# Attention with the values as weights: two output tiles side by side on TensorE, divided by spread inverse row sums on VectorE

## The reference, cut to what matters

```python
# q, k, v: (4 batches, 8 heads, 576, 64)
scores = scale * q @ k.T
thresh = max(scores, axis=-1) - tau
attn   = exp(where(scores >= thresh, scores, -1e9) - max)
attn   = attn / (sum(attn, axis=-1) + 1e-9)
x      = attn @ v                       # heads are joined: x is (4, 576, 512)
# part 2 ("dense" in the kernel), per batch
x_prev = x shifted by one row
xk, xr = mu_k*x + (1-mu_k)*x_prev, mu_r*x + (1-mu_r)*x_prev
x2     = sigmoid(xr @ w_r) * (relu(xk @ w_k)**2 @ w_v)
u      = x2 + real(fft(fft(x2, axis=1), axis=2))
# part 3, over all 2304 rows
out    = u + relu(norm(u) @ w_ch1) @ w_ch2
```

## Time and profile before

| | |
|---|---|
| median of 3 runs | 1061.82 us (1059.22 to 1061.85) |
| the profiled execution | 1060.8 us, its span 1059.0 us |
| granted TensorE clock over the span | 1.00 |
| attention with set-up, nothing beside it | 0 to about 110 us |
| attention with part 2 of the batch before beside it | about 110 to 565 us |
| part 2 of the last batch alone | about 565 to 700 us |
| part 3 | about 700 to 1059 us |

### The profile page before, as it was taken

How to read it: one execution, slowest core, us unless ns; L and a number is a source line. 1 busy time by engine, 2 the same in 40 slices (tenths; PEclk the granted TensorE clock), 3 DMA queues, 4 the chain that set the end, 5 groups by cost and what they waited for, 6 DMA issues and landing times.

```text
span 1059.0 us, 18200 instructions
## 1 busy us (share of the span) xinstructions
PE 1031.8 (97%) x6896; PEld 980.0 (93%) x6896; DVE 580.2 (55%) x1135; ACT 504.4 (48%) x1252; POOL 415.7 (39%) x363
## 2 busy tenths in 40 slices
PE   6899899999999999999999999999999999999998
PEld 6898899999899999999999999888888888888998
DVE  6998995467875467874565687443214214114111
ACT  5989785656775647775647653211111111111110
POOL 4888784334664434573423246331211211111000
PEclk9999999999999999999999999999999999999999
DMA  8736112023302032301023137101001000100000
GB/s 237 203 88 192 45 45 58 3 90 118 102 27 59 1 121 87 105 25 37 20 94 111 45 123 276 41 1 64 9 1 37 36 1 34 38 1 1 36 1 35
DMA packets 41271, 70.08 MB, mean 66 GB/s; under 512 B 6624, under 2 KB 22368, under 8 KB 40672
## 3 DMA queue, kind: packets, MB, share of 16 engines
q1 hardware_dynamic: 40880, 68.59, 20.6%
q10 hardware_dynamic: 304, 0.33, 0.1%
HBM read 56.50 MB, written 12.41 MB: 65 GB/s over the span
## 4 chain that ended last, share of the span: by engine, by line
PE 84%; POOL 5%; DVE 4%; ACT 4%; issue 2%; DMA 0%; SPq 0%; DVEq 0%; POOLq 0%; ACTq 0%
PE PB L840 21%; PE PB L841 21%; PE PB L842 21%; PE PB L906 8%; PE PB L867 6%; PE PB L886 5%; PE PB L908 1%; DVE probs L1443 1%; DVE neg_s L1432 1%; ACT exps L1163 1%; POOL wkl L705 1%; POOL k_lo L696 1%; POOL q_hl L689 1%; ACT mix_v L1235 1%; ACT probsT L1172 1%
## 5 line engine op out<-in xcount | busy, mean ns | idle before, releaser
L1389 ACT ACTIVATE h_hi<-PB 128x464 fp32r<-128x464 f32 (+1 forms) x80 | 44.5, 556 | 329.7 <-PE PB L842 329.7
L1676 DVE SCALAR_TENSOR_TENSOR h_lo<-PB,h_hi 128x464 fp32r<-128x464 f32 (+1 forms) x80 | 51.0, 638 | 256.7 <-ACT h_hi L1389 256.7
L1443 DVE SCALAR_TENSOR_TENSOR probs<-neg_s,thresh,exps 128x576 f32<-128x576 f32 x144 | 158.9, 1104 | 1.6 <-ACT exps L1163 1.3
L906 PE MATMUL PB<-v_sb,probsT 128*128 128x64 f32 (+1 forms) x1152 | 145.9, 270 | 0.0
L906 PEld LDWEIGHTS PB<-v_sb,probsT 128*128 128x128 f32 x1152 | 140.6, 193 | 0.0
L1432 DVE TENSOR_SCALAR_CACHE_REDUCE neg_s<-PB,taus 128x576 f32<-128x576 f32 x144 | 116.9, 812 | 42.5 <-PE PB L867 38.7
L1172 ACT ACTIVATE probsT<-PB 128x256 f32<-128x256 f32 (+1 forms) x288 | 103.5, 414 | 73.2 <-PE PB L886 72.6
L842 PE MATMUL PB<-un_h,w1l 128*128 128x464 f32 (+1 forms) x320 | 118.8, 371 | 0.0
L841 PE MATMUL PB<-h_lo,w2h 128*128 128x464 f32 (+1 forms) x320 | 118.8, 371 | 0.0
L840 PE MATMUL PB<-h_hi,w2h 128*128 128x464 f32 (+1 forms) x320 | 118.8, 371 | 0.0
L842 PE MATMUL PB<-h_hi,w2l 128*128 128x464 f32 (+1 forms) x320 | 118.8, 371 | 0.0
(11 more groups left out here) (204 smaller groups left out, 2432.5 us busy)
## 6 DMA issues: line engine op xcount, KB each, us to landing
q_raw<-qT_dram SPq DMA_DIRECT2D x62, 160.0 KB, 3.1
k_raw<-kT_dram SPq DMA_DIRECT2D x64, 144.0 KB, 3.2
w_raw<-w_dram SPq DMA_DIRECT2D x8, 1024.0 KB, 8.1
u_scr<-x2T SPq DMA_DIRECT2D x4, 1152.0 KB, 4.8
cd<-cd_scr SPq DMA_DIRECT2D x4, 1032.0 KB, 5.0
v_sb<-v_dram SPq DMA_DIRECT2D x16, 256.0 KB, 3.2
u_in<-u_scr SPq DMA_DIRECT2D x4, 928.0 KB, 5.1
out_dram<-u_in SPq DMA_DIRECT2D x16, 232.0 KB, 2.1
```

The lines of the kernel that those rows point to most:

```text
L906: last = nc.tensor.matmul(both[:, own], probsT[:, n % 2, kt * P128:(kt + 1) * P128], v_sb[:, kt, pair % 2, own], start=jj in (0, TAIL) and ...
L1443: nc.vector.scalar_tensor_tensor(probs[:, n % 2, place_of(n):place_of(n) + S], neg_s[:, n % 2, :], thresh[:, col:col + 1], exps[:, n % 2, ...
L1676: nc.vector.scalar_tensor_tensor(h_lo[:, ft % 3, 0:w], bank(4 + ft % 3)[:, 0:w], 0.0, h_hi[:, ft % 3, 0:w].bitcast(F32), ALU.max, ALU.subt ...
```

## The change

- `pv` works on groups: two full tiles of a head, or the mixed tile, or the two last; five groups a pair (slots `jj` 1, 3, 4, 6, 8). The head's values (64 columns) are now the weights, the transposed probabilities move (128 columns). The two tiles of a group go to partitions 0 to 63 and 64 to 127 of one bank, by two matmuls behind each other (`both_halves`). Outputs have channels on the partitions.
- Since rows of queries are now along the free axis, the inverse row sums can't be a scale any more. `spread` lets TensorE multiply `rowinv`, broadcast to 64 columns as weights, with the identity, so that they lie along the free axis on 64 partitions: five pairs of matmuls for a pair of heads. ScalarE copies them to `inv_rows` (`copy_inverse`, two copies a pair), and VectorE multiplies outputs by them into `x_att` (`mixed_out`, one instruction a pair; `tiles_out`, four).
- ScalarE's ten `copy_tile` copies a pair and TensorE's 20 transposes a batch are gone. `xT` is filled from `x_att` in SBUF, by four copies of 576 columns a batch.
- `pv` comes ahead of `transpose_probs` in a slot. The ring of PSUM banks has no groups "x" any more.
- `gate_alone` moves to another place in SBUF.

```diff
+GROUP_OF = (0, 0, 1, 1, 2, 3, 3, 4, 4)
+GROUP_ENDS = {1: 0, 3: 1, 4: 2, 6: 3, 8: 4}
...
+                def both_halves(out, first, second, start, stop):
+                    for half, (weights, moving) in enumerate((first, second)):
+                        last = nc.tensor.matmul(out[half * DH:(half + 1) * DH, :], weights, moving, start=start, stop=stop)
+                    return last
+
+                def spread(pair, tiles, cols):
+                    weights = [rowinv[:, pair % 2, t:t + 1].broadcast_to([P128, DH]) for t in tiles]
+                    moving = [ident[:, :], ident[:, :]] if tiles[0] != tiles[1] else [ident[:, 0:DH], ident[:, DH:P128]]
+                    return both_halves(beside_outputs(pair)[:, cols], (weights[0], moving[0]), (weights[1], moving[1]), True, True)
+
+                def pv_mixed(pair):
...
+                    for kt in range(KT):
+                        weights = [v_sb[:, kt, pair % 2, h * DH:(h + 1) * DH] for h in range(2)]
+                        moving = [probsT[:, n % 2, kt * P128 + h * DH:kt * P128 + (h + 1) * DH] for h in range(2)]
+                        last = both_halves(beside_outputs(pair)[:, 0:DH], (weights[0], moving[0]), (weights[1], moving[1]), kt == 0, kt == KT - 1)
+                    last.then_inc(pv_ready, 1)
+                    pe.wait_ge(inv_ready, pair * 2 + 1)
+                    spread(pair, (TAIL, TAIL), slice(DH, 2 * DH))
+                    for g in range(2):
+                        last = spread(pair, (2 * g, 2 * g + 1), slice(2 * DH + g * P128, 2 * DH + (g + 1) * P128))
+                    last.then_inc(spread_ready, 1)
...
                 def pv(n):
...
                     for kt in range(KT - 1):
-                        last = nc.tensor.matmul(both[:, own], probsT[:, n % 2, kt * P128:(kt + 1) * P128], v_sb[:, kt, pair % 2, own], start=jj in (0, TAIL) and kt == 0, stop=False)
-                    if jj >= TAIL:
-                        last = nc.tensor.matmul(both, probsT[:, n % 2, (KT - 1) * P128:KT * P128], v_sb[:, KT - 1, pair % 2, :], start=False, stop=jj in (TAIL, TILES_PAIR - 1))
+                        weights = v_sb[:, kt, pair % 2, own]
+                        moving = [probsT[:, t % 2, kt * P128:(kt + 1) * P128] for t in tiles]
+                        last = both_halves(outputs(pair)[:, place], (weights, moving[0]), (weights, moving[1]), jj == 1 and kt == 0, False)
+                    if h == 1:
+                        moving = [probsT[:, t % 2, (KT - 1) * P128:KT * P128] for t in tiles]
+                        for head in range(2):
+                            weights = v_sb[:, KT - 1, pair % 2, head * DH:(head + 1) * DH]
+                            place = slice((2 * head + g) * P128, (2 * head + g + 1) * P128)
+                            last = both_halves(outputs(pair)[:, place], (weights, moving[0]), (weights, moving[1]), False, jj == TILES_PAIR - 1 and head == 1)
                     last.then_inc(pv_ready, 1)
+                    if jj == TILES_PAIR - 1:
+                        pe.wait_ge(inv_ready, pair * 2 + 2)
+                        pe.wait_ge(x_out, pair * 5 + 1)
+                        for g in range(2):
+                            last = spread(pair, (TILES_PAIR - 1 - 2 * g, TILES_PAIR - 2 - 2 * g), slice(2 * DH + g * P128, 2 * DH + (g + 1) * P128))
...
                 def dense(d):
-                    for dt in range(DT):
...
-                        for st in range(FULL):
-                            last = nc.tensor.transpose(ring(d, "x", 0, dt)[:, st * P128:(st + 1) * P128], x_att[:, st, dt * P128:(dt + 1) * P128], ident[:, :])
...
+                    if 0 <= n - 4 < TILES:
+                        pv(n - 4)
                     if 0 <= n - 3 < TILES:
                         transpose_probs(n - 3)
-                    if 0 <= n - 4 < TILES:
-                        pv(n - 4)
...
-                def copy_tile(pair, i):
...
+                def copy_inverse(pair, second):
+                    act.wait_ge(spread_ready, pair * 2 + second + 1)
...
+                    nc.scalar.activation(inv_rows[:, to], beside_outputs(pair)[:, source], ACT.Copy).then_inc(inv_copied, 1)
...
-                        nc.scalar.activation(xT[:, dt, 1:FULL * P128 + 1], ring(d, "x", 0, dt), ACT.Copy).then_inc(xt_copied_a, 1)
+                        nc.scalar.activation(xT[:, dt, 1:S + 1], x_att[:, dt, :], ACT.Copy).then_inc(xt_copied_a, 1)
...
+                def mixed_out(pair):
...
+                    nc.vector.tensor_tensor(x_att[:, dt, FULL * P128:S], beside_outputs(pair)[:, 0:DH], inv_rows[:, 0:DH], ALU.mult).then_inc(x_out, 1)
+
+                def tiles_out(pair, h):
...
+                    for odd in range(2):
...
+                        nc.vector.tensor_tensor(to[:, :, odd, :], some[0], some[1], ALU.mult).then_inc(x_out, 1)
...
+                    for at, out_of in ((9, mixed_out), (13, lambda pair: tiles_out(pair, 0)), (14, lambda pair: tiles_out(pair, 1))):
+                        heads, rest = divmod(n - at, TILES_PAIR)
```

More of the change, by code:

```diff
@@ L189, in bank_turns @@
 def bank_turns():
-    order = [(0, "x", 0, i) for i in range(5)]
+    order = []
     for d in range(B):
@@ L207, in bank_turns @@
         d, stage = group[:2]
-        if alone(d) and stage != "x":
+        if alone(d):
             of[group] = next(six)
@@ L211, in bank_turns @@
             of[group] = 4
-        elif alone(d) or (drains(d) and stage == "u"):
+        elif drains(d) and stage == "u":
             of[group] = next(four)
@@ L452, in ring, with outputs, beside_outputs @@
             return bank(BANK_OF[d, stage, c, i])
-        def outputs(pair, i):
-            at = 0 if i == TAIL else i * 2 * DH
-            return bank(6 + (pair + (i == TAIL)) % 2)[:, at:at + 2 * DH]
+        def outputs(pair):
+            return bank(6 + pair % 2)
+        def beside_outputs(pair):
+            return bank(6 + (pair + 1) % 2)
         def mean_out(c):
@@ L898, in pv @@
+                def pv(n):
+                    jj, pair = n % TILES_PAIR, n // TILES_PAIR
+                    if jj not in GROUP_ENDS:
+                        return
+                    if jj == TAIL:
+                        pv_mixed(pair)
+                        return
+                    h, g = half_of(n), row_of(n) // 2
+                    if jj == 1:
                         pe.wait_ge(v_in[pair % 2], 48 * (pair // 2) + 48)
-                    if n == 0:
-                        pe.wait_ge(v_padded, 1)
+                        if pair == 0:
+                            pe.wait_ge(v_padded, 1)
+                        else:
+                            pe.wait_ge(inv_copied, pair * 2)
@@ L901, in pv @@
                     pe.wait_ge(unit_copied, 2 * n + 2)
-                    both = outputs(pair, i)
-                    own = slice(0, 2 * DH) if jj == TAIL else slice(p * DH, (p + 1) * DH)
+                    tiles = (n - 1, n) if h == 0 else (n, n - 1)
+                    own = slice(h * DH, (h + 1) * DH)
+                    place = slice((2 * h + g) * P128, (2 * h + g + 1) * P128)
                     for kt in range(KT - 1):
-                        last = nc.tensor.matmul(both[:, own], probsT[:, n % 2, kt * P128:(kt + 1) * P128], v_sb[:, kt, pair % 2, own], start=jj in (0, TAIL) and kt == 0, stop=False)
@@ L919, in mean @@
                         pe.wait_ge(mean_set, 1)
+                        pe.wait_ge(x_out, B * PAIRS * 5)
                     if c > 0:
@@ L1375, in _ @@
                         copy_units(n - 2)
-                    pair, at = divmod(n - 10, TILES_PAIR)
-                    if 0 <= pair < B * PAIRS:
-                        for i in COPIED_AT.get(at, ()):
-                            copy_tile(pair, i)
+                    for second, at in enumerate((7, 11)):
+                        pair, rest = divmod(n - at, TILES_PAIR)
+                        if rest == 0 and 0 <= pair < B * PAIRS:
+                            copy_inverse(pair, second)
                 def chunk(c, p):
```

127 lines of the change are left out of this document (53 added, 74 removed).

## The result

The changed kernel takes **1068.32 us** (median of 6 runs, 1066.58 to 1070.7) against 1060.0 us (6 runs) of the kernel before beside it: ratio **1.0077, 95% interval 1.0059 to 1.0095**. It is slower by 8 us; the forecast was 1041, 20 us faster. The time lies 0.3 us above the upper end of the range (1068).

What follows compares the result with a forecast made beforehand. TensorE was taken as the bound in most of 110 to 565 us, four engines sharing it from 20 to 100 us. Products -23, transposes -7, VectorE +9, first 100 us 0: -21, so 1041 us, range 1022 to 1068.

Steps and rivals of the forecast that it cites:

- New waits ... Nothing is charged: Waits between engines around the regrouped value product: copies needed are made a slot (some 4 us) before; no time charged.
- The first 100 us. Zero, -4 to +4: Attention with set-up: TensorE and ScalarE lose work, VectorE gains 1.95 us a pair and takes over; zero, -4 to +4.
- The price of a record, 0.060: Value product: moving side by side, loads one by one, 0.060 us a record, 1.9 us less a pair, 23 in all.
- all overlaps: Rival, value product: both halves and their loads overlap, 3.1 us saved a pair instead of 1.9, 1027 us; chance 0.12.
- The drain: Rival, value product: changing the array's division drains it, 60 visits in twelve pairs, 24 us, 1065 us; chance 0.09.
- 33-column rows: Matmuls of 33 columns, followed by 128-column loads 0.12 later as in their own stream: taken as evidence against draining.
- 64-row rows: Transposes of x: going to 64 rows and back, loads start about 0.20 late in, 0.15 out; agrees with draining.
- VectorE, +9: Behind the three changes of batch, where VectorE is the bound: its new work costs 3 us at each, +9 us.
- Transposes, -7: Transposes of x on TensorE go: 9.2 us in all, three batches count, 6.9 us saved.
- Nothing side by side: Rival, value product: the array's halves never run at the same time, 3.0 us more a pair, about 1101 us; chance 0.18.
- late loads: Rival, value product: loads don't go ahead of a waiting matmul, 0.083 us a record, about 1062 us; chance 0.11.
- The stretch of 280 to 418 us: Stretch where TensorE alone is the bound, busy 138.2 of 138.5 us; becoming shorter by some 7 would show the forecast right.

Runs made afterwards that it cites:

- run 3: Kernel before, its own products issued two tiles at a time at the new groups' slots: ahead of the transposes 1083.91 us, behind them 1074.27 us.
- run 1: Changed kernel with TensorE's old order in a slot, transposes of probabilities first, then the value product: 1062.34 us, ratio 1.0024.
- run 4: Changed kernel with TensorE's old order, VectorE's division of the four full tiles cut to 8 of every 128 columns: 1056.69 us, ratio 0.9963.
- run 2: Changed kernel, but in full-tile groups all products of the lower half issued first, then all of the upper half: 1104.38 us, ratio 1.0419.

## Why the prediction was wrong

Sums are for the kernel of which they were made; they are differences of measured times except where a count is named.

| | us |
|---|---|
| kernel before | 1060 |
| two tiles at a time, behind the transposes | +14 |
| the product ahead of the transposes | +10 |
| halves of the array, division on VectorE, no transposes of x | -16 |
| the changed kernel | 1068 |

The last line of the change holds, by counts from the records, -38 for products (12 pairs x 3.2), -7 for the transposes, +18 for visits (below), and a remainder of 11, in which VectorE's new work and the lower clock lie together. Against the forecast of -21 that is 16 us more gained on products, and 24 lost on waits, 18 on visits and 2 in the remainder: within rounding, the +8.

This says what a part costs, and not where. Starts in the profiled executions, in us (single executions, which differ by 3 to 6 us over the whole kernel):

| | exponential of tile 36 | of tile 48 | part 3 |
|---|---|---|---|
| kernel before | 93.4 | 132.4 | 651.0 |
| run 3, grouped, behind the transposes | 96.1 | 135.3 | 663.3 |
| run 3, grouped, ahead of them | 95.4 | 140.7 | 673.9 |
| the changed kernel | 104.4 | 147.0 | 660.8 |
| run 1, the old order | 102.7 | 145.4 | 653.4 |
| run 4, old order, division mostly left out | 99.6 | 140.5 | 645.6 |

- **"New waits ... Nothing is charged": the step that failed most, 24 us with the old products.** "The copy that it needs was made a slot before" was true of slots that are filled with part 2. In the first 110 us a slot is short, and TensorE waited 16.3 us for that copy, though this wait by itself cost little (run 1). The working looked at whom `pv` waits for and never at who waits behind it. `transpose_probs` came later by a whole group; VectorE's mask waits for it (45.3 us in all), then the row maximum, then TensorE. Holding two `probsT` buffers for a group does the same to ScalarE. Run 3 shows 14 + 10 us with the old products, most of it behind tile 48, and run 1 shows 6 for the order in the changed kernel.
- **"The first 100 us. Zero, -4 to +4": 11 us at tile 36.** The bound there was read off the busy shares, and the new one is the ring of waits between the engines. By the table, neither the grouping with the old products (2 to 3 us) nor the order (1.7) makes most of it; leaving out most of the division takes some 3 off. What makes the other 6 (the visits, `spread`, the clock, a longer way through the engines) no run separates: it stays open.
- **The price of a record, 0.060: too high.** It is 0.054 and 0.030, and loads overlap. The rival "all overlaps" was right in its mechanism, and had 0.12. "Loads never run two at a time in the rows of before" was true, but there no two neighbouring loads were for different halves, so these rows could not tell. That gave 12 x 1.3 = 16 us more than forecast.
- **The drain, dismissed on the 33-column rows.** It is there at every visit. In the single records, from start to start, the changed kernel has 222 ns on entering, where the scores' stream of 288 columns goes on after 134, and 153 to the second pair where it is 102 later on. On leaving it has 203 instead of 102, and 165 between the next two transposes instead of 109. Together 0.09 + 0.05 + 0.10 + 0.06 = 0.30 us a visit, 60 visits in the twelve pairs, 18 us (the rival had 24). The rows of 33 columns were nearest in width, but `fp32r`; the 64-row rows, with the product's own type, were nearest in the form of the instruction, and right.
- **VectorE, +9.** The durations were right (421 ns against 0.42). Cutting 16.0 us of it gives 5.6, so all 30 us (64 x 0.421 + 16 x 0.213) would by that share be about 10, if it is even: an estimate, and by it the term is hardly off. But the place is: the table has 5 of the cut's 8 us (in these two executions) ahead of tile 48, where the prediction had 3 of its 9.
- **Transposes, -7.** 64 + 16 records of x are gone, as was forecast; no run tests their price by itself.
- **The lower clock.** Not in the prediction; an estimated 5 to 9 us of the profiled execution, contained in the terms above and not beside them.
- "Nothing side by side" and "late loads" are ruled out by run 2. The forecast's signs that proved right: starts in pairs, loads of 137 to 140 ns, 1.0 us a group, more idle time for row maxima. Its sign of a drain, loads late at each group's edge, came too. The stretch of 280 to 418 us, which was to become shorter by some 7, has the gain as idle time: TensorE has 4.0 us free there where it had 0.3, and from tile 84 to tile 108 it is 107.2 us instead of 109.1.

With the old order of TensorE and VectorE's two copies on GpSimd the change comes to 1060.57, no gain. No version tried here that computes everything beats the kernel before by more than the measurement can tell.

What stays open: how the remainder of 11 us splits between VectorE and the clock, since every run that moves one moves the other; what makes the other half of the first 11 us; and whether deeper `probsT` and `probs` buffers would bring the 14 us of the grouping back.

## What to carry to other kernels

Two float32 products in the two column halves of the array run fully side by side if they alternate in the queue, but count the visits, not only the records: each costs about 0.3 us here, and by this count the visits took back 18 of the 38 us that the products gained. When work is moved or grouped on an engine, ask for everything queued behind it who waits for it and how many buffers it now holds; a version with the old instructions in the new order tells that price by itself, ahead of writing the new ones. Read a suspect's cost by taking it away as well as by doubling it: the two answers here were 0.35 and 0.85 of its own time, the second with a lower clock in it. And look where on the time line a part is lost, not only how much: one table of when the same tile starts in each run would have shown at once that the first tiles and the rest lose by different things. When spread-out work comes out slower, see first who waits for its end.

## What the runs showed of the hardware

- Two weight loads of 64 float32 columns for different halves are under way at one time, mostly 5 to 7 ns apart, beside running matmuls; 128 moving columns then take 109 ns for both halves, where one half alone takes 109 ns in run 2. The Trainium skill (TensorE: Matmul & The Clock Gate, Part 3) gives 2.38 times for three column tiles; here the gain is 2.0 times for two, loads included.
- A change between 128 and 64 columns drains TensorE for a float32 product (load idle for 0.16 us in the value product, 0.32 behind a stream of 464 columns), and not for `fp32r`, whose load starts 2 to 3 ns after the matmul in front has started, as in an unbroken stream.
- A fall of TensorE's granted clock to 0.50 (1.2 GHz) came each time behind a stretch in which TensorE mostly waited, in both kernels; but the same place of the same instructions kept its clock in one execution and lost it in another. Each us at the lower level goes with 0.2 to 0.4 us of time, an estimate from the spread of executions of one kernel.
